# Attention, two mixtures of experts: the order of two groups of transposes, and the place of the row buffers in SBUF

## What is computed

```python
logits = x @ w_gate
e_idx = np.argmax(logits, axis=1)
...
for e in range(E):
    mask = e_idx == e
    ...
    h = np.maximum(x[mask] @ w1[e], 0.0)
    ye = h @ w2[e]
    out[mask] = gate_w[mask, None] * eom[mask, e, None] * ye
```

## The kernel before

| operand | place in 2,048 bytes, from `slot0` |
|---|---|
| expert weights `slots_hi_lo` (both copies), every row of 512 of `w1` and `w2` | 0 |
| `win_hi`, `win_lo`, every row of 512 | 0 |
| `xT_hi`, `xT_lo`, `uT_hi`, `uT_lo`, `rT_hi`, `rT_lo`, `r_sb`, `u_sb` | 0 |
| `wout_hi`, `wout_lo`, moving rows of 264 fp32 (1,056 bytes) one behind another | varies |
| `stage`, `xs`, `xsT_hi`, `xsT_lo` | 128 |

## Time and profile before

### The profile page before, as it was taken

The page is one execution under the profiler, slowest core; times in us unless marked ns, Lnnn a source line. Parts: engine busy times, 40 slices in busy tenths (PEclk is TensorE's granted clock), DMA queues, the critical chain, the costliest instruction groups (busy, mean ns, idle before and its releaser), DMA issues.

```text
span 784.3 us, 16171 instructions
## 1 busy us (share of the span) xinstructions
PE 747.4 (95%) x5536; PEld 648.4 (83%) x5537; DVE 438.1 (56%) x643; ACT 293.1 (37%) x378; POOL 186.1 (24%) x350
## 2 busy tenths in 40 slices
PE   2899999999999999999987999999999999999994
PEld 2799899989989999998876888888888888888883
DVE  5657678787866767677738525313545444444211
ACT  3524434434444443443323435123434434343120
POOL 4002434434311121121112313122221212212121
PEclk9979999999999999999999999999999999999997
DMA  9602442352232223212033614310526162501000
GB/s 318 236 1 68 153 131 94 108 172 95 67 123 77 67 90 111 67 67 80 15 135 147 257 42 141 134 53 21 186 95 230 66 241 70 221 22 53 12 27 21
DMA packets 22923, 84.60 MB, mean 108 GB/s; under 512 B 4078, under 2 KB 4334, under 8 KB 20976
## 3 DMA queue, kind: packets, MB, share of 16 engines
q1 hardware_dynamic: 16944, 67.46, 24.1%
q0 software_dynamic: 5952, 16.79, 6.8%
HBM read 73.48 MB, written 13.89 MB: 111 GB/s over the span
## 4 chain that ended last, share of the span: by engine, by line
PE 88%; DVE 6%; issue 2%; ACT 1%; DMA 1%; SPq 0%; POOL 0%; DVEq 0%; POOLq 0%; ACTq 0%
PE banks L1070 72%; PE banks L1215 3%; PE banks L1101 3%; PE banks L1091 3%; PE banks L1120 2%; PE banks L1083 2%; PE banks L1192 2%; PE banks L1142 1%; DMA stage<-w_both 1%; DVE prob L775 1%; DVE ssum L769 1%; DVE stat L796 1%; ACT uT_hi L626 1%; DVE uT_lo L779 0%; DVE hmax L783 0%
## 5 line engine op out<-in xcount | busy, mean ns | idle before, releaser
L1070 PE MATMUL banks<-slots_hi_lo,rT_hi 128*128 128x512 f32 x464 | 149.0, 402 | 0.0
L1070 PE MATMUL banks<-slots_hi_lo,xsT_hi 128*128 128x512 f32 x464 | 127.4, 397 | 0.3 <-issue 0.3
L1070 PEld LDWEIGHTS banks<-slots_hi_lo,xsT_hi 128*128 128x128 f32 x464 | 87.3, 189 | 20.4 <-issue 0.5
L1070 PEld LDWEIGHTS banks<-slots_hi_lo,rT_hi 128*128 128x128 f32 x464 | 83.4, 190 | 14.8
L1070 PE MATMUL banks<-slots_hi_lo,rT_lo 128*128 128x512 f32 x232 | 91.3, 393 | 0.0
L546 POOL DMA_INDIRECT out<-ys,rows_out x29 | 29.6, 1020 | 251.1 <-DVE ys L1041 251.1
L1070 PE MATMUL banks<-wout_hi,uT_hi 128*128 128x264 f32 x384 | 82.7, 296 | 3.2 <-DVE uT_lo L779 3.2
L659 ACT ACTIVATE r_sb<-banks 128x1024 f32<-128x1024 f32 x29 | 29.7, 1025 | 136.1 <-PE banks L1070 136.1
L1070 PE MATMUL banks<-wout_hi,uT_lo 128*128 128x264 f32 x384 | 77.9, 284 | 0.0
L1070 PE MATMUL banks<-wout_lo,uT_hi 128*128 128x264 f32 x384 | 77.8, 284 | 0.0
L921 DVE TENSOR_TENSOR rT_lo<-banks,rT_hi 128x1024 fp32r<-128x1024 f32 x29 | 35.5, 1225 | 75.6 <-ACT rT_hi L665 75.6
(11 more groups left out here) (175 smaller groups left out, 1188.0 us busy)
## 6 DMA issues: line engine op xcount, KB each, us to landing
raw_w<-experts SPq DMA_DIRECT2D x14, 2048.0 KB, 7.3
k_sb<-k_win SPq DMA_DIRECT2D x24, 384.0 KB, 3.5
v_sb<-v_win SPq DMA_DIRECT2D x24, 384.0 KB, 4.6
q_sb<-q_t SPq DMA_DIRECT2D x24, 256.0 KB, 2.7
x_rows<-x SPq DMA_DIRECT2D x24, 256.0 KB, 2.0
stage<-experts POOLq DMA_DIRECT2D x8, 512.0 KB, 5.9
stage<-w_both SPq DMA_DIRECT2D x4, 512.0 KB, 6.2
wout_t<-w_out_t SPq DMA_DIRECT2D x1, 2048.0 KB, 12.1
```

The source lines that it names most:

```text
L1070: ins = mm(o, lhs, rhs(part, k, n), start=(k == first and lhs is not None and part == 0 and parts == (0, 1)), stop=(k == final and parts = ...
```

## The change

It has two parts. In `step_c` of PE, `xs_turn(t + 1)` moves from ahead of the second product to directly ahead of `r_turn(t)`, and the second product is cut after 5 of its 8 chunks in place of 4. In the layout, `stage` (and with it `xs` and `xsT`) moves up to the next place that is a multiple of 2,048 bytes from `slot0`, which is 1,920 bytes further on. No instruction is added or removed.

```diff
         x2 = [ra.take(f"x2_{n}", [P, YW], F32) for n in range(2)]
+        ra.at += (slot0 - ra.at) % (4 * BANK)
         stage_at = ra.at
         stage = [ra.take(f"stage{n}", [P, CH], F32) for n in range(2)]
...
             def step_c(t):
                 hidden(t, range(KD))
+                expert_out(t + -1, range(0, 5))
                 xs_turn(t + 1)
-                expert_out(t + -1, range(0, KF // 2))
                 r_turn(t)
-                expert_out(t + -1, range(KF // 2, KF))
+                expert_out(t + -1, range(5, KF))
```

## The result

The changed kernel took 782.83 us in the median of its first 4 runs (781.2 to 784.3), beside 787.73 us for the kernel before (787.34 to 788.48). The ratio is 0.9936, with an interval from 0.9915 to 0.9957: faster, by 4.9 us or 0.64%. The forecast was 783.6 us with a range from 782.8. By the ratio the time is 787.82 x 0.9936 = 782.78 us, just past the range's lower end; by the interval of the ratio it lies between 781.1 and 784.4. The profiled execution took 781.2 us.

A forecast was written before the change was run, and what follows sets the result against it. PE's busy time was taken to bound the kernel; 0.10 (tile 0), 0.14 (tile 1), 4.55 (steps 2 to 27) and -0.56 (step 28) give 4.2 us less, 787.82 to 783.6 us, range 782.8 to 786.0.

The forecast's parts named there:

- the 0.4 us for the scatter of the runs: Whole run: allowance of 0.4 us for scatter, included in the main case's own range of 782.8 to 784.6 us.
- The place of the buffers: `hidden` in the tile loop: with `xsT` at place 0, each matmul goes from 0.2325 to 0.2267 us, 0.14 us a tile.
- The rival that the place has no part: `hidden` keeps its pace whatever its operand's place; time 787.6 us, no measurable change; chance 13%.
- the half case: `hidden`'s pace falls only part of the way, 0.07 us a tile; time 785.6 us; chance 6%.
- the bad one: Rival: loads and moving rows collide at equal places, so `hidden` gets slower; time 791.6 us; chance 4%.
- The order of the transposes: Tile loop step: joining two transpose blocks saves 0.035 us a step, bounded by 0.01 and 0.05.
- one loss of 0.10 to 0.12: Matmuls behind the joined 12 transposes: one slow restart in us, replacing losses of 0.12 and 0.10 behind two blocks.
- The end of the loop: Last `expert_out(28)`: PE waits for `rT_lo` with 9 matmuls ahead in place of 12; 0.7 us lost, once.
- Tiles 0 and 1: Tiles ahead of the loop: `hidden`'s faster pace gives 0.10 us in tile 0 and 0.14 us in tile 1.
- The waits: Tile loop: split rows reach `hidden` in time, margin 0.75 us; ACT, DVE and GpSimd waits put at nothing.
- the 0.108 us for a transpose: Transposes from `xs` and `r_sb`: both read as 0.108 us each more, so speaking neither for nor against the place.
- The sum: Whole kernel: tile 0 0.10, tile 1 0.14, steps 2 to 27 4.55, step 28 -0.56; 4.2 us less.

The follow-up runs named there:

- e1: Only the new place of `stage`, `xs` and `xsT`, old order of transposes, against the kernel before: 782.62 us, ratio 0.9948.
- e3: The changed kernel again, new place and new order together, against the kernel before: 783.45 us, ratio 0.9960.
- e2: Only the new order in `step_c`, old place of the buffers, against the kernel before: 787.21 us, ratio 1.0005.
- e13: e9 once more, only `xs` and `xsT` moved and `stage` left, five rounds against the kernel before: 782.34 us, ratio 0.9948.
- e14: e1 once more, `stage`, `xs` and `xsT` all moved, five rounds against the kernel before: 783.37 us, ratio 0.9955.
- e8: e1 with `rT`, `r_sb` and `ys` moved on by 128 bytes, so the unequal place falls to the second product: step 12.380 us.
- e5: e1 with `stage` and row buffers at 512 bytes in place of 0: step 12.253 us, tile 0 to the end 379.2 us.
- e12: e1 with dense output weight rows at multiples of 256 bytes, against the kernel before: 781.88 us, ratio 0.9935.
- e4: The changed kernel with the second product cut after 4 of 8 chunks, against the kernel before: 782.83 us, ratio 0.9942.
- e6: e1 with `stage` and row buffers at 256 bytes in place of 0: step 12.253 us, tile 0 to the end 379.3 us.
- e9: e1 with `stage` left at 128, only `xs` and `xsT` moved: step 12.253 us, tile 0 to the end 379.3 us.
- e10: e1 with everything from the first weights buffer on moved 128 bytes up: step 12.267 us, tile 0 to the end 379.8 us.
- e11: e1 with `xs` left at 128 and `xsT` at 0: step 12.267 us, tile 0 to the end 379.6 us.
- e7: e1 with `stage` and row buffers at 64 bytes in place of 0: step 12.407 us, tile 0 to the end 383.7 us.

## Why the prediction was right, and where it failed

Two terms failed. The one that put the result outside the range is the 0.4 us for the scatter of the runs. The one that made the sum too large is the gain of the new order, 0.035 us a step. The mechanism that carries the change, the place, was right. From tile 0 on, where the whole forecast of 4.2 us lies, the profiles show 3.6, and a lead of 1.2 us that no edit made came on top; that the total of 4.9 is so near to 4.2 is luck.

- **The place of the buffers** (0.14 us a tile): right, to the hundredth. `hidden` takes 5.44 us, and the fast pace of the earlier trace rows was the right one to take. The rival that the place has no part is refuted by e1, the half case too, and the equal place is not the bad one. The Trainium skill (TensorE: Matmul & The Clock Gate, Step-by-step: what each phase is for) says that loading the next tile's weights takes no SBUF read bandwidth from the running matmul. By that alone the place should not matter, and these runs do not agree: with a weight load beside each matmul, they show 0.0058 us more a matmul where the two operands lie 128 bytes apart, and nothing at 256. Whether it is the load's reads that cost it was not measured, and no run has these matmuls without a load beside each.
- **The order of the transposes** (0.035 us a step, bounds 0.01 to 0.05): the step that failed. Measured is 0.006 (e3 against e1) and 0.000 (e2 against before), under the lower bound. The two losses did become one, but "one loss of 0.10 to 0.12" was a little more: the nine matmuls take 2.164 us where 9 x 0.2267 is 2.04. The joined transposes take 1.232 us, where the two blocks had taken 0.357 + 0.790 = 1.147 (means of 25 steps, e1 for the old order): 0.085 more, and the prediction had reckoned 1.22 - 1.15 = 0.07. This alone eats most of the 0.098 us that were lost behind the second block. And the products ahead give a little back: 3.41 for 15 in place of 3.40, and the first matmul of `hidden`, 0.004 over the steady pace. The difference of two numbers rounded to 0.01 us was taken as a gain and multiplied by 26. It made 0.9 us of the 4.2, where 0.15 came.
- **The end of the loop** (0.70 us lost): right, 0.6. DVE ended `rT_lo` at 763.11, 2.65 us after the transposes (760.46), and PE began 0.05 later. The 0.1 us that the prediction added for starting again behind a wait did not come.
- **Tiles 0 and 1** (0.24 us): right. Between the transposes of tile 0 and `hidden(2)` 32.28 us passed and now 31.98, 0.30 less (31.92 in e3, 32.05 with the place only).
- **The waits** put at nothing were nothing. The rows came 1.4 us ahead of `hidden` in every step from step 3 on, where a margin of 0.75 had been worked out, on the safe side.
- **A reading that shows less than it says:** the 0.108 us for a transpose came from (0.79 - 0.36) / 4, one block from `xs` and one from `r_sb`, so it could not compare the two. Start by start in the trace, they follow one another after 0.108 to 0.109 us in both blocks.
- **The sum**: with the order at its measured value and the end at 0.6, the terms give 3.6 us, which is what the profiles show from tile 0 on and what e3 measured (0.9960, 3.2 us, with an interval from 1.7 to 4.6).
- **The scatter** ("0.4 us for the scatter of the runs") is why the first result lay below the range although the sum had promised too large a gain. It was read off three runs within 0.84 us, while 28 runs of the same kernel on another chip reached over 6.4 us. The first profile of the changed kernel had 1.22 us ahead of tile 0 that no edit explains, and its four runs reached over 3.1 us. The interval of the first result alone reaches 1.6 us to either side; the range should have reached as far around the forecast. That the lead is no effect of the place of `stage` is what e13 and e14 show: with `stage` left where it was, tile 0 begins at 399.9 us, and with it moved at 402.3.

## What to carry to other kernels

Where the loads of the stationary operand lie under a dense stream of fp32r matmuls, compare the pace of groups of one shape before anything else; a group that is some per cent slower than its like, with no wait, may owe it to the place of its operand in SBUF, and a multiple of 256 bytes between the two operands cured it here for the price of a little padding. On matmuls of 512 columns it was worth 2.5% of their pace, on those of 264 columns, whose places had varied, 1.4%. Joining blocks of transposes gave nothing, and cutting a product short ahead of the last wait cost 0.6 us. A gain that is the difference of two rounded rows is no gain before it is larger than their rounding.

## What the runs showed of the hardware

**The start scatters with the granted clock.** The table of 36 to 56 us holds a stretch at the half level (1.2 GHz), whose length differs between executions. The last three numbers of a row are the mean granted clock, the DMA share and GB/s. In order: before, the changed kernel, cut after 4, and `xsT` at 64.

```profile
36.00:56.00 20.00, 20.00 (x111) 18.55 (x111) 11.24 (x19) 5.08 (x8) 1.91 (x8) 0.74 0.00 0
```

```profile
36.00:56.00 20.00, 19.97 (x123) 18.34 (x123) 11.70 (x19) 5.79 (x10) 1.91 (x8) 0.83 0.00 0
```

```profile
36.00:56.00 20.00, 20.00 (x97) 18.40 (x97) 10.93 (x19) 4.50 (x8) 1.92 (x8) 0.66 0.00 0
```

```profile
36.00:56.00 20.00, 20.00 (x94) 18.30 (x93) 8.67 (x14) 5.01 (x8) 1.91 (x8) 0.61 0.02 6
```

All sixteen profiles are in the next table. Some have a second stretch at the half level, shortly ahead of tile 0, and its column is the mean granted clock from 390 to 410 us:

| 36 to 56 us | 390 to 410 us | tile 0 begins at, us |
|---|---|---|
| 0.83 | 1.00 | 399.9 (changed), 399.9 (e13) |
| 0.83 | 0.91 | 401.2 (e3) |
| 0.74 | 1.00 | 401.1 (before), 400.5 (e8) |
| 0.74 | 0.91 | 401.8 (e2), 402.0 (e5), 402.3 (e14), 400.8 (e12, 1.3 us of it by its even rows) |
| 0.66 | 0.91 | 403.5 (e1), 404.2 (e4), 404.6 (e6), 402.4 (e9), 403.7 (e10), 404.3 (e11) |
| 0.61 | 0.91 | 407.2 (e7) |

PE is busy through the first stretch in all of them (at least 19.9 of 20 us); in the 26 us at the start, while the weights are loaded, it was busy for 8.5 us in the kernel before (second number behind 0.00:26.00):

```profile
0.00:26.00 26.00, 8.53 (x112) 7.34 (x114) 14.33 (x17) 8.67 (x10) 10.36 (x12) 1.00 0.95 344
```

The second stretch, in the changed kernel and in e3, which is the same kernel:

```profile
396.50:400.00 3.50, 3.18 (x26) 3.18 (x27) 0.35 (x2) 0.00 (x0) 0.32 (x2) 1.00 0.20 78
```

```profile
396.50:400.00 3.50, 3.20 (x15) 3.21 (x15) 0.34 (x2) 0.00 (x0) 0.24 (x2) 0.51 0.16 61
```

In the 3.5 us ahead of it PE was busy for 1.45 and 1.43 us, and only in e3 did the clock fall. Up to 383 us the two profiles run alike (the first product of the last block begins at 383.06 and 383.03 us), so the 1.36 us between them at tile 0 arise here.

The less time at the full level, the later all that follows. No edit stands behind it: the changed kernel and e3, and e9 and e13, are the same kernels and begin tile 0 at 399.9 and 401.2, and at 402.4 and 399.9 us. The times of whole runs go with it: of the 28 runs of the kernel before, the longest (791.07 us) has the lowest mean granted clock, 0.977, and the two with the highest, 0.988, took 784.84 and 784.87. What decides the stretches was not found.

**The loss behind transposes hardly depends on their number.** In the old order it was 0.12 us behind 4 transposes and 0.10 behind 8; behind 12 it was 0.12 to 0.13, whether 9 or 12 matmuls followed. Start by start in the traces (means of 25 steps) the transposes of a block follow one another after 0.109 us, the next matmul begins only 0.028 us after the last of them, and the one behind it 0.314 to 0.318 us later, where the steady pace is 0.227. So about 0.09 us of the loss falls on that one matmul, and 0.08 us are about what the last transpose is short of (0.109 - 0.028). In a joined block the transpose that had been the last of its own block takes its full 0.109, and this gives back most of what one loss less saves.
